# Attention in a fused kernel: values of a unit in front of the scores of the unit three ahead

## The reference

```python
scores = scale * np.matmul(q, k.transpose(0, 1, 3, 2))
keep = is_sink | in_window            # 4 sinks, window of 128
a = softmax of np.where(keep, scores, -1e9)
x = np.matmul(a, v), laid out as (3072, 512)
...
out[mask] = gate_w[mask, None] * (np.maximum(x[mask] @ w1[e], 0.0) @ w2[e])   # for each expert e
...
out = np.maximum(np.maximum(x @ w1, x @ w2), x @ w3) @ w_out
```

## Time and profile before

| | |
|---|---|
| runs shown | 998.23, 998.23, 996.86 us; median 998.23 |
| the profiled execution | 996.38 us |
| its span, first to last instruction | 994.7 us |
| TensorE busy | 948.0 us (95%) |
| VectorE, ScalarE, GpSimd busy | 403.9, 313.7, 95.4 us |
| steady attention units on TensorE | from about 22 to 234 us |
| mean granted TensorE clock | 0.99 |

### The profile page before, as it was taken

One profiled execution on the slowest core, in us unless ns is written; L12 is line 12 of the kernel. 1 busy time (PEld: TensorE's weight loads), 2 busy tenths in 40 slices (PEclk: granted clock), 3 DMA queues, 4 the chain that ended last, 5 costly groups with the idle time before them and its releaser, 6 DMA issues.

```text
span 994.7 us, 15555 instructions
## 1 busy us (share of the span) xinstructions
PE 948.0 (95%) x5140; PEld 749.3 (75%) x5140; DVE 403.9 (41%) x1308; ACT 313.7 (32%) x759; POOL 95.4 (10%) x175
## 2 busy tenths in 40 slices
PE   3999999998899999999999949999999999999998
PEld 2677666665478888888888838888888888888887
DVE  4778686776452222622222673303213124032120
ACT  2676666764411111411111441211211212112111
POOL 2112213130200000000000050100100100000000
PEclk9999999999999999999999979999999999999999
DMA  4345655371551111341111040010200200100001
GB/s 104 125 160 178 216 169 185 103 255 53 181 212 42 47 48 42 116 137 42 42 42 42 30 139 1 26 60 1 64 21 0 84 0 0 42 1 21 23 1 42
DMA packets 35955, 76.99 MB, mean 77 GB/s; under 512 B 7488, under 2 KB 9536, under 8 KB 35904
## 3 DMA queue, kind: packets, MB, share of 16 engines
q1 hardware_dynamic: 22016, 49.55, 14.6%
q0 software_dynamic: 6080, 19.93, 6.5%
q10 hardware_dynamic: 7808, 6.87, 2.2%
HBM read 52.74 MB, written 23.59 MB: 77 GB/s over the span
## 4 chain that ended last, share of the span: by engine, by line
PE 70%; DMA 1%; POOL 0%; issue 0%; DVE 0%; ACT 0%; ACTq 0%; DVEq 0%; POOLq 0%
PE bank L652 22%; PE bank L654 22%; PE bank L653 22%; PE bank L681 2%; PE bank L762 1%; PE bank L647 1%; POOL yr L488 0%; DMA yr<-y_sorted,pos_out 0%; DMA y_sorted<-y 0%; DVE y L1435 0%; DVE yT_lo L1512 0%; DVE xT_lo L1417 0%; ACT yT_hi L1007 0%; ACT o_sb L1028 0%; DVE yr L1505 0%
## 5 line engine op out<-in xcount | busy, mean ns | idle before, releaser
L654 PE MATMUL bank<-yT_hi,m_lo 128*128 128x512 f32 x432 | 168.1, 389 | 0.0
L820 ACT ACTIVATE probs<-masked,row_min 128x264 f32<-128x264 f32 (+1 forms) x192 | 93.4, 487 | 80.3 <-DVE row_min L1089 79.4
L652 PE MATMUL bank<-yT_hi,m_hi_b 128*128 128x512 f32 x288 | 112.0, 389 | 0.0
L653 PE MATMUL bank<-yT_lo,m_hi_b 128*128 128x512 f32 x288 | 112.0, 389 | 0.0
L1533 DVE TENSOR_TENSOR b_sb<-bank,a_sb 128x512 f32<-128x512 f32 x36 | 24.9, 691 | 187.8 <-PE bank L654 187.8
L654 PEld LDWEIGHTS bank<-yT_hi,m_lo 128*128 128x128 f32 x432 | 81.1, 188 | 16.8
L1013 ACT ACTIVATE gT_hi<-g_sb 128x512 fp32r<-128x512 f32 x36 | 22.7, 632 | 200.1 <-DVE g_sb L1536 200.1
L1089 DVE CUSTOM_DVE_ANT_0 masked<-bank,masks 128x264 f32<-128x264 f32 (+1 forms) x192 | 70.5, 405 | 27.9 <-PE bank L510 26.8
L510 PE MATMUL bank<-kT,qT 64*128 64x264 f32 (+2 forms) x384 | 67.0, 428 | 13.3 <-issue 11.8
L652 PE MATMUL bank<-w_hi,xT_hi 128*128 128x512 f32 x192 | 76.7, 399 | 1.1 <-DVE xT_lo L1417 1.0
L652 PE MATMUL bank<-w_hi,hT_hi 128*128 128x512 f32 x192 | 75.8, 395 | 0.0
(11 more groups left out here) (209 smaller groups left out, 1544.0 us busy)
## 6 DMA issues: line engine op xcount, KB each, us to landing
w_sb<-in_moe_w SPq DMA_DIRECT2D x6, 2048.0 KB, 10.5
xr<-x_sorted POOLq DMA_DIRECT2D x28, 256.0 KB, 3.0
y_sorted<-y ACTq DMA_DIRECT2D x26, 256.0 KB, 2.0
kT<-in_k_t SPq DMA_DIRECT2D x16, 400.0 KB, 4.1
qT<-in_q_t SPq DMA_DIRECT2D x16, 384.0 KB, 3.1
v_in<-in_v_p SPq DMA_DIRECT2D x16, 384.0 KB, 3.0
out<-o_sb SPq DMA_DIRECT2D x24, 256.0 KB, 2.0
m_sb<-in_moe_w SPq DMA_DIRECT2D x6, 768.0 KB
```

The lines of the kernel that those rows point to most:

```text
L652: pe.matmul(psum, a_hi, b_hi, start=first, stop=False)
L653: pe.matmul(psum, a_hi, b_lo, start=False, stop=False)
L654: return pe.matmul(psum, a_lo, b_hi, start=False, stop=last)
L820: last = act.activation(probs[n % 2][:, hd, 0:win_of(t)], masked[n % 2][:, hd, 0:win_of(t)], ACT.Exp, bias=row_min[:, n % 2, hd:hd + 1], s ...
```

## The change

The values of unit n go in front of the scores of unit n+3 in TensorE's program. The signal that a pair's qT and kT may be overwritten moves by one unit, so that it still comes from a product issued behind the pair's last scores. Nothing changes on the other engines.

```diff
@@ values(n)
-                        if w == hd == 0 and (n + 3) % QT == QT - 1:
+                        if w == hd == 0 and (n + 2) % QT == QT - 1:
 
                             mm.then_inc(qk_free, 1)
@@ TensorE's loop over n
                     sinks(n)
+                    values(n)
                     if n + 3 < NUNITS:
                         scores(n + 3)
-                    values(n)
```

## The result

The changed kernel took 1034.15 us (median of 4 runs, 1032.79 to 1034.88) against 997.55 for the kernel before (4 runs beside it): +36.6 us, a ratio of 1.0366 with a 95% interval of 1.0348 to 1.0384. The forecast was 1035, slower, by one mechanism. The profiled execution took 1034.78 us around a span of 1033.2.

What follows compares the result with a forecast made beforehand. Attention ran at TensorE's pace, 12.74 us per six units; a chain over TensorE and VectorE would make it 15.22. 38.4 - 1.4 = +37.0 us gave 1035 us on the median's scale, range 1023 to 1048.

Steps and rivals of the forecast that it cites:

- The chain: Attention: loop over TensorE and VectorE through masks and oT copy takes 15.22 us per six units against 12.74, +38.4 us.
- Values to scores: TensorE's distance from values to scores, taken as 0.59 us; ends 0.42 and 0.68, or -15.8 and +8.4 us.
- What was already lost: Attention: waits for oT already in the trace are part of the new ones; 1.4 us taken off.
- the ranks' wait: TensorE's wait for rank products, once a batch, released by VectorE after its copy: stays, 1.5 us in all.
- VectorE's own work: Routing pieces between oT copies, at most 1.71 us, fit the waiting time: no cost, under 5 us if that fails.
- the signal: SP's signal freeing qT and kT comes one unit later; loads still arrive in time: costs nothing.
- ScalarE's cover: Attention: pT is kept 0.99 us before the earlier values need it, exponentials have longer units: nothing paid.
- The clock did not fall: Rival: stalls lower TensorE's clock in attention; +150, 1148 us for good, or 1090 if half the time; chance 0.04.
- the scores of 1.25 us at 22.99: Sign for the clock falling: early scores took 1.25 us against 0.72, nearer the pace of 1.2 GHz than 2.4.
- the masks stay covered: Rival: attention's masks remain covered and load idle shrinks, 16 us less, 982 us; chance 0.02.
- only part is exposed: Rival: weight loads fill in on both sides in attention, so +15, 1013 us; chance 0.08.
- Filling the stall from behind: TensorE pulls only weight loads ahead and keeps matmuls in order, so transposes can't be moved into the stall.

Runs made afterwards that it cites:

- experiment 1: Changed kernel with VectorE's copy of oT of unit n in front of both masks of unit n+3: 997.26 us against 996.23 for the kernel before.
- experiment 2: Changed kernel with VectorE's copy of oT between the two masks instead of behind both: 1011.68 us against 996.23 for the kernel before.
- (3): Changed kernel with an extra 0.22 us VectorE copy and its wait in each unit, between the masks and the oT copy: 1055.51 us.
- experiment 5: Changed kernel with the extra 0.22 us VectorE copy and its wait as the first thing of each unit: 1033.69 us.
- (9): Kernel before with only the signal that frees qT and kT one unit later: 998.84 us against 997.24.
- experiments 4 and 6: Changed kernel with additions ahead of the masks: in 4 an extra VectorE copy and its wait, 1045.09 us; in 6 only a redundant wait, 1044.26 us.
- experiment 10: Kernel before with the sink product behind the scores of n+3 instead of in front: 1004.29 us against 997.0.

## Why the prediction was right

**The chain** (its part 1). Right in kind and size: 15.22 forecast for six units, 15.23 measured, with each term in place. Taking the masks off the chain (experiment 1) takes the loss off, taking one of the two off leaves less than half of it (15.4 of 36.6 us, experiment 2), and time added to the chain comes through in full (3). A stall is shown here as the difference of two lengths, 1.79 for the answer and 1.38 for TensorE's cover.

**Values to scores** (part 2), the one unknown with wide ends, was 0.59, the nearest row. The 0.17 us of weight-load idle stands after values in both orders, ahead of transposes in the old one and of scores in the new one.

**What was already lost** (part 3). 1.4 us were taken off; it was about 3.4. 38.4 were worked out for 93 units and the stage grew by 35.0. The starts of the row products, unit by unit in both traces, show where. A steady pair takes 2.49 us more, and the growth is smaller in two kinds of places, by about 1.5 us each. The first are units in which the kernel before has late oT copies or other delays already (n = 2, 6, 60, 84, 85); these are what the 1.4 stood for, and it was right for them. The second are the three stretches around the ranks' wait (n = 32 and 33, 56 and 57, 80 to 82), which the prediction kept as a term of its own beside 93 full stalls: VectorE reads the ranks behind its copy of oT in its program, so the unit behind that wait finds oT copied and has no stall (n = 33 takes 2.17 us in both kernels, where the same kind of unit grows by 0.52 in other pairs), and the ranks' own wait grew less than that, from 1.5 to 2.5 us in all three. So this term was too small by some 2 us. It nearly cancels against an unforeseen 1.6 us, by which the medians rise behind attention. The forecast's nearness, 1035 against 1034.15, is luck in its last two microseconds. The 1.6 us can't be assigned: the swings of the clock behind idle stretches are as large.

**VectorE's own work, ScalarE, the signal** (parts 3 to 5). Costed at nothing and shown so: 0.22 us more work in each unit at VectorE's idle place added nothing (5); no wait of the values for pT is among the changed kernel's waits; the signal alone moves the time by 0.08%, inside its interval (9). ScalarE's cover was the least safe of these: the prediction read it for pT, in one unit, and passed over the exponentials with a word. It holds in the changed kernel, where one matmul waits 0.5 us for exponentials and the units have become longer. Where they are short again (1, 2), ScalarE is the next wait.

**The rivals.** The clock did not fall: 1.00 granted over the six units, and in units with a stall of 0.46 us at the weight loads (0.25 at the matmuls) the values behind it take 0.66 us and the scores 0.72, as before. One sign that the prediction gave for this rival is not borne out: it took the scores of 1.25 us at 22.99 for the pace of the lower clock, but the profile of the kernel before has a granted clock of 1.00 from 20 to 26 us. What slowed them stays open, and so does the 1148 us that was worked out from them. The Trainium skill, "TensorE: Matmul & The Clock Gate", section "A second HAM failure mode: psum-queue depth-cycling", tells of a kernel in which short idles between groups of matmuls made the clock swing; this trace does not show that, with the granted clock at 1.00 over 15.23 us. That the masks stay covered, and that only part is exposed, fell with the 15.23.

**Filling the stall from behind.** In none of the 85 waits of weight loads for oT does a product of a later step come early: the steps of TensorE follow each other in the program's order from one end of the stage to the other. The Trainium skill, "TensorE: Matmul & The Clock Gate", section "Step-by-step: what each phase is for", says that TensorE moves only weight loads ahead; the trace agrees.

## What to carry to other kernels

When steps of one engine are reordered, follow each result to the engine that answers and read what stands in front of it there: the loop's length is the sum around both engines, and it is to be set against the work that the first one has in the meantime (1.79 against 1.38 here). An engine that idles 1.4 us a unit can still be the one that all wait for, if its queue has the wrong step in front. In the kernel before, the covers fit by hundredths of a microsecond, and none of the five reorderings run here was faster: the change itself, the copy first in each of the two TensorE orders, the copy between the masks, the sinks behind the scores. Three of them moved the last wait to ScalarE. That they did not pay says nothing of orders that were not run.

## What the runs showed of the hardware that was not expected

A redundant wait in front of an instruction that waits anyway is not free. The second wait, satisfied long before, made the mask start 0.86 us behind the scores instead of 0.75 (experiments 4 and 6), 0.11 us a unit and 10 us over the stage, though VectorE was idle at the time. In experiment 5 the added wait stands where VectorE idles before its next mask, and the time did not change; whether it costs 0.11 us there too, hidden by the idle time, that run can't tell.

A sink product whose weights are loaded only after its own wait, or behind the scores, takes 0.42 us to the next step (122.50 to 122.92 in the changed kernel, 122.26 to 122.68 in experiment 10), and 0.32 where they are loaded under the row product (120.53 to 120.85 in the kernel before). The order of steps thus changed TensorE's pace with no matmul waiting for another engine in those six units: 12.74 to 13.40 us for the same 112 matmuls.
